# Attention scores per head with high and low queries stacked on all rows, and a second PSUM bank for hidden products

## The reference

```python
# 1: attention on the 32 largest scores of a row
scores = q @ k.T / sqrt(64)                      # per batch and head, 576 x 576
kth = 32nd largest score of each row
attn = softmax(where(scores >= kth, scores, -1e9))
x = (attn @ v), heads side by side               # 4 x 576 x 512
# 2: gated projection
gate = sigmoid(causal convolution of x over 5 tokens, per channel)
y = (gate * (x @ w_val)) @ w_out
# 3: Fourier mixing and a feed-forward part
u = y + real(fft over tokens of fft over channels of y)
out = u + relu(layernorm(u) @ w_ch1) @ w_ch2     # 512 -> 2048 -> 512
```

## Time and profile before

| | |
|---|---|
| runs (3) | median 1088.55 us, 1085.76 to 1089.21 |
| the profiled execution | 1087.9 us, of it the span of the program 1085.7 us |
| TensorE busy | 994.5 us, 92% of the span |
| VectorE busy | 830.2 us, 76% |
| ScalarE busy | 624.0 us, 57% |
| GpSimd busy | 333.7 us, 31% |
| scores' matmuls (L541) | 762 on 64 rows beside 6 of tile 1; the left-over tiles' (L534) 96 on 128 rows |

### The profile page before, as it was taken

The page is one execution under the profiler, slowest core; times in us unless marked ns, Lnnn a source line. Parts: engine busy times, 40 slices in busy tenths (PEclk is TensorE's granted clock), DMA queues, the critical chain, the costliest instruction groups (busy, mean ns, idle before and its releaser), DMA issues.

```text
span 1085.7 us, 19701 instructions
## 1 busy us (share of the span) xinstructions
PE 994.5 (92%) x6848; PEld 779.3 (72%) x6848; DVE 830.2 (76%) x1804; ACT 624.0 (57%) x1349; POOL 333.7 (31%) x474
## 2 busy tenths in 40 slices
PE   5876777899999999999999999999999999999997
PEld 3454555676688887766777888766778887668896
DVE  7999999898999997969988877889998953120000
ACT  5888678555676766546666665556666662122211
POOL 2575353022332222123322213133322222243221
PEclk9987768899999999999999999999999999999999
DMA  7466546112267776212667464321466674239874
GB/s 224 158 196 197 175 166 228 53 40 70 100 212 264 251 280 224 85 29 57 240 212 274 160 224 172 104 62 50 173 228 232 248 259 155 78 117 359 298 247 131
DMA packets 78113, 190.91 MB, mean 176 GB/s; under 512 B 9408, under 2 KB 27584, under 8 KB 78016
## 3 DMA queue, kind: packets, MB, share of 16 engines
q1 hardware_dynamic: 77872, 189.41, 50.9%
q10 hardware_dynamic: 144, 0.26, 0.1%
HBM read 168.14 MB, written 21.50 MB: 175 GB/s over the span
## 4 chain that ended last, share of the span: by engine, by line
PE 74%; DVE 12%; ACT 7%; issue 5%; DMA 0%; POOL 0%; ACTq 0%; DVEq 0%; POOLq 0%
PE p_m L707 17%; PE p_m L722 17%; PE p_m L581 12%; PE p_t L570 8%; PE p_t L554 7%; DVE rest L926 6%; PE p_s L541 5%; DVE top L932 4%; PE p_m L611 3%; ACT prob L799 2%; ACT pT L813 2%; PE p_m L601 2%; PE p_t L574 1%; DVE top L917 1%; PE p_m L646 1%
## 5 line engine op out<-in xcount | busy, mean ns | idle before, releaser
L932 DVE MAX8 top<-rest 128x8 f32<-128x576 f32 x432 | 304.3, 745 | 0.0
L926 DVE MATCH_REPLACE8 rest<-top,rest 128x576 f32<-128x576 f32 x288 | 211.5, 741 | 0.0
L1140 POOL TENSOR_TENSOR hid_lo<-hid,hid_hi 128x256 fp32r<-128x256 f32 (+1 forms) x128 | 104.8, 818 | 339.4 <-ACT hid_hi L872 339.2
L722 PE MATMUL p_m<-w_st,hid_hi 128*128 128x512 f32 x576 | 182.7, 398 | 0.4 <-POOL hid_lo L1140 0.4
L707 PE MATMUL p_m<-un_hi,w_st 128*128 128x256 f32 (+1 forms) x1024 | 165.3, 304 | 13.5 <-ACT hid_hi L872 13.5
L788 ACT ACTIVATE s_all<-p_s 128x576 f32<-128x576 f32 x143 | 92.5, 647 | 122.3 <-PE p_s L541 103.3
L707 PEld LDWEIGHTS p_m<-un_hi,w_st 128*128 128x128 f32 x1024 | 142.3, 189 | 26.3 <-issue 23.5
L554 PE MATMUL p_t<-id_sb,prob 128*128 128x128 f32 x720 | 117.0, 295 | 34.9 <-ACT prob L805 34.5
L871 ACT ACTIVATE hid<-p_m 128x256 f32<-128x256 f32 (+1 forms) x128 | 51.3, 400 | 137.4 <-PE p_m L707 137.3
L570 PE MATMUL p_t<-pT,v_sb 128*64 128x128 f32 (+1 forms) x1600 | 110.1, 289 | 17.3 <-ACT pT L813 17.3
L554 PEld LDWEIGHTS p_t<-id_sb,prob 128*128 128x128 f32 x720 | 82.1, 147 | 60.1 <-ACT prob L805 40.2
(11 more groups left out here) (107 smaller groups left out, 1481.8 us busy)
## 6 DMA issues: line engine op xcount, KB each, us to landing
w_st<-w_split SPq DMA_DIRECT2D x256, 512.0 KB, 4.5
w_split<-w_st SPq DMA_DIRECT2D x32, 512.0 KB, 3.0
u<-w_ch SPq DMA_DIRECT2D x32, 256.0 KB, 3.8
k_raw<-kT SPq DMA_DIRECT2D x16, 288.0 KB, 3.2
v_sb<-v SPq DMA_DIRECT2D x16, 256.0 KB, 3.5
wslot<-w_val SPq DMA_DIRECT2D x4, 1024.0 KB, 5.3
wslot<-w_out SPq DMA_DIRECT2D x4, 1024.0 KB, 5.2
out<-u SPq DMA_DIRECT2D x16, 256.0 KB, 2.5
```

The lines of the kernel that those rows point to most:

```text
L722: mm = pe.matmul(mbank(j), h[i % 2][:, P * j:P * j + P], w2_st[i % NB2][:, w, :], start=f == 0 and part == 0, stop=f == FC - 1 and part == 2)
L926: dve.match_replace(rest[tt % 2][:, :], top[tt % NK][:, 8 * n - 8:8 * n], src, LOWEST).then_inc(s_chain, 1)
L932: found = dve.max(top[tt % NK][:, 8 * n:8 * n + 8], rest[tt % 2][:, :])
L1140: pool.tensor_tensor(hid_lo[i % 2][:, 0:width(b, g)], hid[:, 0:width(b, g)], hid_hi[i % 2][:, 0:width(b, g)].bitcast(F32), ALU.subtract).t ...
```

## The change

- `scores`: a regular tile now is 128 rows of **one** head against all 576 keys. For each head there is a query tile `q_st[h]`, whose one half of the partitions holds `hi` and the other `lo` of the same head, and key tiles `k_hi[h]`, `k_lo[h]`, in which the head's keys stand twice, on partitions 0 to 63 and 64 to 127. A matmul on all 128 rows sums both halves, so a tile is two key halves times (k_hi, k_lo), four matmuls. The left-over tile runs both heads' query blocks, eight matmuls. Its low-low product is included.
- The left-over tile is last in every pair, so the units of odd pairs end one slot later or earlier than before.
- Queries and keys are loaded per head, each twice (both partition halves), at tile 8 (head 0 of pair p + 2) and tile 4 (head 1 of pair p + 1); `hi` copies and `lo` parts are made per head at the ends of slots given by `HIGH_Q`, `HIGH_K`, `LOW_Q`, `LOW_K`. Pair 0's head 1 is loaded into two idle `x_new` buffers.
- Score tiles have six buffers `s_sb` in place of room for eight; tile 1 uses `p_s` like all others and waits for tile 0's copy.
- `hidden_bank(b, g, f)` alternates banks 2 and 3 for f = 1 and for f from 12 on in ch0, and throughout ch1 of even batches; `hidden(i)` waits for the last eviction of the same bank.
- `z_last` is a view of `hid`.

```diff
-        q_hi = [sb(f"q_hi{i}", [P, QW], F32R) for i in range(2)]
-        q_lo = [sb(f"q_lo{i}", [P, QW], F32R) for i in range(2)]
-        k_hi = [sb(f"k_hi{i}", [P, S], F32R) for i in range(2)]
-        k_lo = [sb(f"k_lo{i}", [P, S], F32R) for i in range(2)]
+        q_st = [[sb(f"q_st{h}{i}", [P, SP], F32R) for i in range(2)] for h in range(2)]
+        k_hi = [[sb(f"k_hi{h}{i}", [P, S], F32R) for i in range(2)] for h in range(2)]
+        k_lo = [[sb(f"k_lo{h}{i}", [P, S], F32R) for i in range(2)] for h in range(2)]
...
+def hidden_bank(b, g, f):
+
+    if g == 0:
+        return 3 if f == 1 or f >= 12 and f % 2 == 0 else 2
+    return 2 if b % 2 == 0 and f % 2 else 3
...
-LOAD_AT = 7
-HIGH_Q, LOW_Q, HIGH_K, LOW_K = 0, 1, 2, 3
-HIGH_Q0, LOW_Q0, HIGH_K0, LOW_K0 = 2, 3, 4, 5
+LOAD = {8: 0, 4: 1}
+HIGH_Q, HIGH_K, LOW_Q, LOW_K = {0: 0, 5: 1}, {1: 0, 6: 1}, {2: 0, 6: 1}, {3: 0, 7: 1}
+HIGH_Q0, HIGH_K0, LOW_Q0, LOW_K0 = {2: 0, 6: 1}, {3: 0, 6: 1}, {3: 0, 7: 1}, {4: 0, 7: 1}
...
+                def load_qk(p, h):
+                    if h:
+                        if p:
+                            sp.wait_ge(s_lo[0], 2 * (p + 1))
+                    elif p == 1:
+                        sp.wait_ge(s_lo[0], 2)
+                    elif p:
+                        sp.wait_ge(s_lo[1], 3 * p)
+                    q, k = raw(p, h)
                     b, p = divmod(p, PAIRS)
+                    for half in range(2):
+                        rows = slice(D * half, D * half + D)
+                        sp.dma_start(q[rows, :], qT[b, 2 * p + h]).then_inc(s_qk_in[h], 16)
+                        sp.dma_start(k[rows, :], kT[b, 2 * p + h]).then_inc(s_qk_in[h], 16)
...
                 def scores(t):
                     p, i = tile_of(t)
-                    if i == TILES - 1:
-
-                        for o in range(2):
-                            for n, (q, k) in enumerate(terms):
-                                mm = pe.matmul(bank[:, o, 0:HALF_S], q[:, WHOLE:QW], k[:, o * HALF_S:o * HALF_S + HALF_S],
-                                               start=n == 0, stop=n == 2)
-                    else:
-                        o, c0 = i % 2, P * (i // 2)
-                        for n, (q, k) in enumerate(terms):
-                            for h in range(2):
-                                at = slice(D * h, D * h + D)
-                                mm = pe.matmul(bank[:, h, 0:HALF_S], q[at, c0:c0 + P],
-                                               k[at, o * HALF_S:o * HALF_S + HALF_S], start=n == 0, stop=n == 2)
+                    heads = [0, 1] if i == TILES - 1 else [i % 2]
+                    for h in heads:
+                        pe.wait_ge(s_lo[h], (2 + h) * (p + 1))
+                    if t:
+                        pe.wait_ge(s_copy, t)
+                    cols = slice(P * (i // 2), P * (i // 2) + P)
+                    for o in range(2):
+                        parts = [(h, k[h][p % 2]) for h in heads for k in (k_hi, k_lo)]
+                        for n, (h, k) in enumerate(parts):
+                            mm = pe.matmul(p_s[:, o, 0:HALF_S], q_st[h][p % 2][:, cols],
+                                           k[:, o * HALF_S:o * HALF_S + HALF_S], start=n == 0,
+                                           stop=n == len(parts) - 1)
                     mm.then_inc(s_qk, 1)
...
                     pe.wait_ge(m_w1in[i % NB1], 16 * (i // NB1 + 1))
-                    if i:
-                        pe.wait_ge(m_hev, i)
+                    if hidden_before(i) is not None:
+                        pe.wait_ge(m_hev, hidden_before(i) + 1)
+                    if g == 0 and f == 12:
+                        pe.wait_ge(m_unT, 2 * NR * (b + 1))
...
+                    if h == 0:
+                        act.activation(q[:, 0:S], src, ACT.Copy).then_inc(s_hi, 1)
+                    else:
+                        act.activation(q[:, 0:whole], src[:, 0:whole], ACT.Copy).then_inc(s_hi, 1)
+                        act.activation(q[:, whole + REST:SP], src[:, whole:S], ACT.Copy).then_inc(s_hi, 1)
```

More of the change, by code:

```diff
@@ L20 @@
 TAPS = 5
-FILLS = 15
+NS = 6
+FILLS = 18
 TOPK = 32
@@ L44 @@
 XW = TAPS - 1 + S
-NU = 4
-WHOLE = (S // P) * P
-QW = WHOLE + P
 HALF, HALF_S = 256, S // 2
@@ L93, in un_cols, with hidden_before @@
     return slice(c0, c0 + ROWS[r][1])
-HIDDEN_BANK = [2, 3]
+def hidden_bank(b, g, f):
+    if g == 0:
+        return 3 if f == 1 or f >= 12 and f % 2 == 0 else 2
+    return 2 if b % 2 == 0 and f % 2 else 3
+def hidden_before(i):
+    place = [hidden_bank(j // FC // 2, j // FC % 2, j % FC) for j in range(i + 1)]
+    return max((j for j in range(i) if place[j] == place[i]), default=None)
 VAL_BANK = [3, 0, 1, 2, 3, 0, 1, 2]
@@ L218, in build @@
         z = sb("z", [P, 2, DM])
-        z_last = sb("z_last", [P, NCOS])
         ab = sb("ab", [P, DM])
@@ L226, in build @@
         hid = sb("hid", [P, WIDEST])
+        z_last = hid[:, 0:NCOS]
         hid_hi = [sb(f"hid_hi{i}", [P, WIDEST], F32R) for i in range(2)]
@@ L252, in build @@
         s_feat_ev = sem("s_feat_ev")
-        s_q_in = sem("s_q_in")
-        s_k_in = sem("s_k_in")
+        s_qk_in = [sem(f"s_qk_in{h}") for h in range(2)]
         s_v_in = [sem(f"s_v_in{i}") for i in range(2)]
-        s_qhi = sem("s_qhi")
-        s_khi = sem("s_khi")
-        s_lo = sem("s_lo")
+        s_hi = sem("s_hi")
+        s_lo = [sem(f"s_lo{h}") for h in range(2)]
         s_qk = sem("s_qk")
@@ L474, in step @@
                                     sp.dma_start(out[bb, c0:c0 + m, :], u_row(bb, r)).then_inc(m_put, 16)
-                load_keys(0)
-                sp.wait_ge(s_zero, 1)
-                load_left_queries(0, sp)
+                for half in range(2):
+                    sp.dma_start(k_raw[D * half:D * half + D, :], kT[0, 0]).then_inc(s_qk_in[0], 16)
+                load_qk(0, 1)
                 sp.wait_ge(s_zero, FILLS)
@@ L494, in _ @@
                     p, i = divmod(s, TILES)
-                    if i == LOAD_AT and p + 2 < ALL_PAIRS:
-                        load_queries(p + 2)
-                        load_keys(p + 2)
+                    ahead = p + 2 - LOAD.get(i, 0)
+                    if i in LOAD and ahead < ALL_PAIRS:
+                        load_qk(ahead, LOAD[i])
                     i = part_due(s, 1)
@@ L778, in copy_scores, with high_keys @@
+                def high_keys(p, h):
+                    act.wait_ge(s_qk_in[h], 64 * (p + 1))
+                    act.activation(k_hi[h][p % 2][:, :], raw(p, h)[1], ACT.Copy).then_inc(s_hi, 1)
                 def copy_scores(t):
-                    i = tile_of(t)[1]
                     act.wait_ge(s_qk, t + 1)
-                    if t >= 2 * NU and (t % 2 == 0 or i == TILES - 1):
-                        act.wait_ge(s_drop, (t // 2 - NU) * 2 + 2)
-                    bank = p_m[:, 0:2 * BANK].rearrange("p (o n) -> p o n", o=2) if t == 1 else p_s
@@ L869, in step @@
                         act.wait_ge(m_h, i + 1)
-                        bank = mbank(HIDDEN_BANK[g], width(b, g))
+                        bank = mbank(hidden_bank(b, g, n), width(b, g))
                         act.activation(hid[:, 0:width(b, g)], bank, ACT.Relu).then_inc(m_hf, 1)
                         act.activation(hid_hi[i % 2][:, 0:width(b, g)], bank, ACT.Relu).then_inc(m_hev, 1)
-                act.dma_start(q_raw[:, 0:WHOLE], qT[0, 0:2, :, 0:WHOLE].rearrange("h d n -> (h d) n")).then_inc(s_q_in, 16)
-                high_keys(0)
-                high_queries(0)
+                for half in range(2):
+                    act.dma_start(q_raw[D * half:D * half + D, :], qT[0, 0]).then_inc(s_qk_in[0], 16)
+                high_keys(0, 0)
+                high_queries(0, 0)
+                high_queries(0, 1)
+                high_keys(0, 1)
                 for s in plan:
@@ L1043, in _ @@
                         select(s - SELECT - 1, 2)
+                    p, h = split_at(s, LOW_Q0, LOW_Q) or (0, 0)
+                    if p > POOL_PAIRS and h == 1:
+                        low_queries(p)
+                    p, h = split_at(s, LOW_K0, LOW_K) or (0, 0)
+                    if p > POOL_PAIRS and h == 1:
+                        low_keys(p)
                     for b, c, taps in conv_due(s):
@@ L1064, in reciprocal @@
                     pool.wait_ge(s_exp, t + 1)
[L1065 to L1067 removed]
+                    if n >= 5:
+                        pool.wait_ge(s_pv, n - 4)
+                    i = tile_of(t)[1]
+                    c = slice(i - i % 2, i + 1)
                     pool.tensor_scalar(rinv[:, c], psum_row[:, c], EPS_SUM, 2.0, ALU.add, ALU.mult).then_inc(s_radd, 1)
                     pool.wait_ge(s_radd, n + 1)
[L1070 removed]
+                    pool.tensor_tensor(rinv[:, c], rinv[:, c], power[:, 1:2 + i % 2], ALU.pow).then_inc(s_rinv, 1)
                 def scale_out(t):
```

170 lines of the change are left out of this document (80 added, 90 removed).

## The result

The changed kernel takes 1068.27 us (median of 4 runs, 1067.29 to 1069.93); the kernel before takes 1087.15 on the same chip. The ratio is 0.9827, 95% interval 0.9805 to 0.9850: 18.9 us or 1.7% faster. I had said 1077, with a sum of 10.9 us for the gain and a range from 1068 to 1093. The forecast's own range, 1070 to 1083, did not hold, and over two fifths of the gain were not in the sum.

The account below looks back on a forecast made before the run. VectorE was taken to set the pace until 215 us, TensorE after. Scores -11.3, banks -6, start +1.4, ScalarE and POOL +2, VectorE +3 sum to -10.9 us on 1087.9, giving 1077 us, range 1068 to 1093.

Parts of the forecast that it names:

- The forecast's own range: Whole kernel at 1070 to 1083 us, from changes of -18.6 and -5; given a chance of 0.50.
- scores on TensorE: Score tiles from 215 us on: full-row one-head tiles take 118.5 us instead of 129.8, -11.3 us (-5 to -14).
- ScalarE and POOL: Per-head copies at slot ends: ACT charged +1.5 us (0 to +10), POOL +0.5 (0 to +3).
- VectorE lets it through: TensorE's gain must come out of VectorE's room of 91 us, 43.7 of it exponent waits; charged +3 us (0 to +12).
- hidden banks: Hidden products using the other bank skip waits for the previous eviction, -6 us (-3 to -8.7).
- start: First batch: more loads and copies, second tile without its own bank, VectorE's later start carried; +1.4 us (0 to +3).
- order of the tiles: Left-over rows last, attention units shifted by a slot in odd pairs; counted only in the scores, no term of its own.
- the rules weighed ahead: Score matmuls: changing tiling mode drains TensorE (for the change); row tiles run concurrently for about one's price (against it).
- the rival by which the split form is the cheaper way: Score tiles: gaps belong to semaphore waits and stay, so scores cost +14.8 instead of -11.3, 1103 us; chance 0.10.
- The charges for ScalarE, POOL and VectorE: Added copies at slot ends and VectorE's limited room: ACT +1.5 us, POOL +0.5, VectorE +3.
- the ten waits of the earlier trace: TensorE's waits for the hidden eviction that the change can remove, 8.7 us together, first 1.98 us, last 0.90.
- more than forecast: Rival: no charge for VectorE, ACT or POOL, all hidden waits gone, TensorE's other waits shrink; about 1067 us, chance 0.10.

Follow-up runs that it names:

- experiment 5: Changed kernel with eight memsets of a scratch tile on VectorE ahead of the first MAX8; 1072.56 us, ratio 0.9865.
- Experiments 1 and 2: Changed kernel with six full-row matmuls in a one-head tile instead of four, 1092.84 us; kernel before with four split pairs a regular tile instead of three, 1097.94 us.
- experiment 1: Changed kernel with six full-row matmuls in a one-head tile instead of four; 1092.84 us, ratio 1.0058.

## Why the prediction was right, and where its sum was not

Taking parts of the change away one at a time splits the 18.9 us. Putting the order back costs 5.2, taking the banks away 4.3; the start costs 2.5, measured at VectorE's first MATCH_REPLACE8 and carried as experiment 5 tells. What remains is -18.9 + 5.2 + 4.3 - 2.5 = -11.9 us for the scores and everything that I had charged beside them. This is a remainder and not a measurement: the parts overlap, and with the banks at their 7.8 us alone it would be -8.4.

| step | predicted | measured |
|---|---|---|
| scores on TensorE | -11.3 | remainder, with the next two rows: -11.9 |
| ScalarE and POOL | +2.0 | in the row above |
| VectorE lets it through | +3.0 | in the row above |
| hidden banks | -6 | -4.3 on top, -7.8 alone |
| start | +1.4 | +2.5 |
| order of the tiles | 0 | -5.2 |
| sum | -10.9 | -18.9 |

**Scores: the mechanism and the prices of a tile were right.** 1.076, 1.276 and 1.604 us were worked out from the left-over tile; the trace shows 1.07, 1.28 and 1.61. The count was a little off: in the trace 28 tiles from slot 44 on stand behind an attention product, and not 23. With the median of each kind of tile, TensorE's time for them falls from 129.7 to 119.5 us, 10.2 less and not 11.3. Experiments 1 and 2 show what such time is worth: from slot 44 to slot 143 two more full-row matmuls a tile cost 17.6 us for 23.2 worked out, one more split pair 8.7 for 11.6, three quarters both times. That all of experiment 1's 24.6 us come near 23 is luck, since 7.9 of them arose before slot 44, where the sum counts nothing. For the rules weighed ahead: the drain at a change of tiling mode in the Trainium skill (TensorEngine Tiling (Array Packing), Key Properties) and the concurrency of row tiles (TensorE: Matmul & The Clock Gate, Part 3) both agree with the traces (0.24 and 0.22 us beside the pairs, 0.13 to 0.14 for a pair); 0.21 us a tile is what is left between them in this stream (1.28 - 1.07), and the rival by which the split form is the cheaper way is out.

**The charges for ScalarE, POOL and VectorE: too high, by how much is not settled.** By the remainder of -11.9 against -11.3 nothing of my +5 us is left, and this mis-sizing is 5 of the 8 us that the sum missed. The trace points the same way: from slot 44 to slot 143 TensorE's idle time fell by 3.5 us, and no wait for these engines grew by more than 1.4. ScalarE's doubled copies are there, 50 with 29.1 us of durations in that stretch for 20 with 14.1, but its busy time grew only from 411.6 to 415.5 us, because the evictions of transposes now overlap more with what stands beside them (their part of the busy time is 59.4 us for 66.3). Against it stand the three quarters of experiments 1 and 2: by them 11.3 us on TensorE would be worth 8.5 (an estimate), so some of what I charged may have been paid. VectorE, with 46 us idle in that stretch, let most of the gain through.

**The order of the tiles: the step that failed.** I wrote that attention units are "shifted by a slot in odd pairs", counted what that does to the scores behind an attention, and costed the shift itself at nothing. It is worth 5.2 us in the changed kernel, nearly all of it at a single place: slots 40 to 42, at the end of the first batch's attention. Against the kernel before 3.6 us of that are seen at this place, after what the other parts cost there. In a list of 144 slots I looked at the average slot, and not at the one hand-over where the bound passes from VectorE to TensorE and every operation of TensorE counts in full.

**The start: right mechanism, +2.5 for +1.4,** inside its 0 to +3. **The banks:** -4.3 for -6, inside -3 to -8.7; the ten waits of the earlier trace rows were counted as the kernel before has them, and with the rest of the change fewer are there to take (8.5 us for 13.5 over the whole execution). By the table the prediction missed 5.0 (charges) + 0.6 (scores) + 5.2 (order) of the gain and had 1.7 (banks) and 1.1 (start) too much of it: 8.0 us.

The median lies nearer to the rival "more than forecast" (about 1067) than to the forecast. Of its reasons the missing charges fit in part; the waits on the hidden eviction did not all go (5.9 us are left over the whole execution), and the order of the tiles was not among them. That the number still lies in the stated range is luck.

What stays open: what moved the granted clock between the two orders, so how much of the order's 5.2 us is the clock and how much the place of the units (the changed kernel with the left-over tile first has no trace with another clock there); how the remainder of 11.9 us divides between scores and charges; and, as said, whether an earlier start would pay.

## What to carry to other kernels

- Before packing small contractions on half of TensorE's rows, price the tile from the end of what goes before to the end of what comes behind. Here three split pairs in a stream of full-row matmuls cost nearly as much as six full-row ones (1.28 us for 1.35); stacking the high and low parts to fill all rows needed only four.
- A kernel that passes from one bounding engine to another has a hand-over, and work on the chain there counts in full. Look at what the change moves in exactly those slots, also where it only reorders. Here the gain came out of the first engine's wait for the second, 4.1 us before the change and 0.5 after it.
- Parts of one change overlap, so a remainder is not a measurement of the last part. Measured alone a part can be worth nearly twice what it is worth on top of the others.

## What the runs showed of the hardware that was not expected

Entering and leaving the split form costs nearly as much as three full-row matmuls, with three pairs as with four: four pairs take 1.42 us and three 1.28, so by that slope of 0.13 us no pairs at all would leave 0.89, where four full-row matmuls in 1.07 leave 0.54. The difference is 0.35 us a tile. It can be found again in the rows, where a split tile is set against a full-row one: 0.08 us ahead of the first pair (0.32 for 0.24 between starts), 0.11 behind it (0.24 for 0.13), 0.09 ahead of the transposes (0.22 for 0.13) and 0.06 in them (0.77 for 0.71). And with the tiles in another order the granted clock from 196 to 206 us was 0.96 in place of 0.75.
